# A retention layer feeding a mixture of experts on one core: four-quarter state products, one mask product and a new order inside a chunk

## What is computed

```python
B, H, S, D = 2, 8, 768, 64
gamma = 1.0 - 2.0 ** (-5.0 - arange(H))
for t in range(S):                                   # retention, per batch and head
    state = gamma * state + outer(k[t], v[t])        # D x D
    y[t] = 1/sqrt(D) * (q[t] @ state)
x = y with the heads side by side                    # (B, S, 512)
logits = x @ w_gate; local = sigmoid(x @ w_local)    # 8 experts
e = argmax(logits[s]) if s == 0 or local[s] < 0.5 else e of the token before
out[s] = softmax(logits[s])[e] * (relu(x[s] @ w1[e]) @ w2[e])      # F = 1024
```

## Time and profile before

| | us |
|---|---|
| median of 3 runs | 260.91 (260.75 to 261.23) |
| the profiled execution | 260.31 |
| its span (first to last instruction) | 258.6 |
| PE busy | 248.3 |
| DVE busy | 194.4 |
| ACT busy | 133.6 |
| POOL busy | 62.2 |

### The profile page before, as it was taken

How to read it: one execution, slowest core, us unless ns; L and a number is a source line. 1 busy time by engine, 2 the same in 40 slices (tenths; PEclk the granted TensorE clock), 3 DMA queues, 4 the chain that set the end, 5 groups by cost and what they waited for, 6 DMA issues and landing times.

```text
span 258.6 us, 5040 instructions
## 1 busy us (share of the span) xinstructions
PE 248.3 (96%) x1932; PEld 214.9 (83%) x1932; DVE 194.4 (75%) x426; ACT 133.6 (52%) x254; POOL 62.2 (24%) x57
## 2 busy tenths in 40 slices
PE   7899999999899999999999999999999999999991
PEld 3688888887788888988988898898899889889891
DVE  2445999997986895999798688858869868886700
ACT  1313537537468473557438457545845844764310
POOL 0563343442002423004301600510240061011011
PEclk9999999999999999999999999999999999999998
DMA  6999999962201837556908835771791785440000
GB/s 205 372 380 413 414 411 413 429 246 74 91 0 42 308 124 228 208 175 228 376 18 326 332 150 203 290 310 38 316 392 56 284 314 202 160 203 13 0 38 13
DMA packets 11387, 56.83 MB, mean 220 GB/s; under 512 B 1751, under 2 KB 2135, under 8 KB 9570
## 3 DMA queue, kind: packets, MB, share of 16 engines
q1 hardware_dynamic: 7056, 45.96, 45.8%
q0 software_dynamic: 2560, 7.34, 8.1%
q10 hardware_dynamic: 1746, 3.19, 3.3%
HBM read 50.20 MB, written 7.34 MB: 223 GB/s over the span
## 4 chain that ended last, share of the span: by engine, by line
PE 75%; DVE 12%; DMA 6%; ACT 2%; issue 2%; POOLq 0%; SPq 0%; DVEq 0%
PE ps L1271 18%; PE ps L1290 10%; PE ps L1292 10%; PE ps L1291 10%; PE ps L1273 9%; DMA x_gathered<-x_rows,gather_idx 4%; PE ps L1158 3%; PE ps L1170 3%; PE ps L1251 2%; DVE scores_masked L824 2%; DVE w_split L837 2%; PE ps L1314 2%; PE ps L1203 2%; PE ps L1193 2%; ACT slot_values L549 2%
## 5 line engine op out<-in xcount | busy, mean ns | idle before, releaser
L1271 PE MATMUL ps<-x_sorted_T,w_split 128*128 128x240 f32 (+6 forms) x288 | 84.5, 362 | 0.2 <-DVE x_sorted_T L851 0.2
L1273 PE MATMUL ps<-x_sorted_T,w_split 128*128 128x120 f32 (+6 forms) x288 | 72.7, 252 | 0.0
L844 DVE TENSOR_TENSOR w_split<-w_raw,w_split 128x1024 fp32r<-128x1024 f32 x56 | 66.2, 1220 | 8.2 <-ACT w_split L555 8.2
L555 ACT CAST w_split<-w_raw 128x1024 fp32r<-128x1024 f32 x56 | 55.8, 1041 | 6.5 <-DMA w_raw<-w 6.5
L1271 PEld LDWEIGHTS ps<-x_sorted_T,w_split 128*128 128x128 f32 x288 | 54.1, 188 | 4.2 <-issue 0.7
L1273 PEld LDWEIGHTS ps<-x_sorted_T,w_split 128*128 128x128 f32 x288 | 54.9, 191 | 0.3
L858 DVE TENSOR_REDUCE h_sums<-ps 128x120 f32<-128x240 f32 (+6 forms) x72 | 40.3, 561 | 19.2 <-PE ps L1273 18.4
L565 ACT ACTIVATE hT<-h_sums 128x120 fp32r<-128x120 f32 (+6 forms) x72 | 26.0, 365 | 52.2 <-DVE h_sums L858 52.1
L1290 PE MATMUL ps<-w_split,hT 128*128 128x512 f32 x120 | 48.3, 402 | 0.0
L1292 PE MATMUL ps<-w_split,hT 128*128 128x512 f32 x120 | 47.4, 395 | 0.0
L1291 PE MATMUL ps<-w_split,hT 128*128 128x512 f32 x120 | 47.4, 395 | 0.0
(11 more groups left out here) (146 smaller groups left out, 272.8 us busy)
## 6 DMA issues: line engine op xcount, KB each, us to landing
w_raw<-w SPq DMA_DIRECT2D x14, 2048.0 KB, 9.4
qkv_sb<-qkv SPq DMA_DIRECT2D x22, 512.0 KB, 13.5
w_raw<-w SPq DMA_DIRECT2D x8, 512.0 KB, 16.4
x_rows<-x_rows_sb ACTq DMA_DIRECT2D x12, 256.0 KB, 6.5
qkv_sb<-qkv SPq DMA_DIRECT2D x2, 256.0 KB, 14.5
x_gathered<-x_rows,ident_and_w_router POOLq DMA_INDIRECT x12, 8.5
out<-y_rows,ident_and_w_router POOLq DMA_INDIRECT x12, 5.2
c_route_sb<-c_route SPq DMA_DIRECT2D x1, 152.0 KB, 10.5
```

Of the source, the lines that this page charges most:

```text
L555: nc.scalar.copy(ws[:, par, 0, half, at:at + PIECE], raw[:, half, at:at + PIECE]).then_inc(w_hi_rdy[half], 1)
L844: V.tensor_tensor(ws[:, par, 1, half, at:at + PIECE], raw[:, half, at:at + PIECE], ws[:, par, 0, half, at:at + PIECE].bitcast(fp32), ALU.s ...
L1271: MM(at[:, 0:2 * w].rearrange("p (a t) -> p a t", a=2), ws[:, par, 0, 0, cols], xTs[:, k, :, sub], start=(k == 0), stop=(k == KD - 1), ski ...
L1273: last = MM(at[:, w:2 * w], ws[:, par, 1, 0, cols], xTs[:, k, 0, sub], start=False, stop=(k == KD - 1), skip_group_check=True)
```

## The change

1. `from_state` gives the four 64 by 64 quarters of the array work: row half r takes its head's input as before, and the pair's number n (even or odd) picks the output's partition half. The outputs of the two row halves go to two banks (3 and 4, columns 256 to 511 of each; 0 and 1 for the last chunk). Heads thus stand in another order in x (HEADS), and the host puts the rows of the router and of w1 into the same order.
2. `from_chunk` is cut in two halves by r. The first half (r = 1) goes before `from_state`, the second (r = 0) behind it.
3. `state_products` moves ahead of both, and so waits for the last `state`; `state(m)` on DVE now waits until `from_state(m)` has read the old state (new semaphore `fs_done`).
4. The outputs share bank 3 with the transposed rows, so `from_state(m)` waits until ACT has copied the rows of chunk m - 1 (`xr_ready`). The rows and logits are laid out at steps of 175 columns across banks 2 and 3.
5. `masked` is one instruction of 1024 columns over banks 0 and 1. Just before it DVE raises a new semaphore (`masking`), for which POOL's `k_decayed` of the same chunk waits.
6. ACT's `e0_high` goes behind `logits_out` and `rows_out`. DVE's `e0_low` goes behind `state` in chunks with m % 3 = 2, and behind the router's part at the end of the iteration in the others.

PE's order in iteration m becomes: `qk(m + 1)`, `rows_and_logits(m - 1)`, `to_col`, `state_products(m)`, `from_chunk(m, 1)`, `to_rows`, `table`, `rank`, `from_state(m)`, `from_chunk(m, 0)`. For m = 11 `from_state` and `from_chunk(m, 1)` stand ahead of `rows_and_logits(10)`.

```diff
+HEADS = [0, 2, 4, 6, 1, 3, 5, 7]
+XL_AT, XL_STEP = 25, 175
...
-        y_ps = [bank(n).rearrange("p (n t) -> p n t", n=HP) for n in (4, 1)]
+        xl_ps = bank(2, 2)[:, XL_AT:XL_AT + HP * XL_STEP].rearrange("p (n w) -> p n w", n=HP)
+        y_ps = [bank(n, 2).rearrange("p (r w) -> p r w", r=2)[:, :, 2 * P:4 * P] for n in (3, 0)]
...
+                pool.wait_ge(masking, m + 1)
                 nc.gpsimd.tensor_tensor(
                     kd[:, m % 2, :, :], io[:, s, 2, :, :].rearrange("p n (h d) -> p (n h) d", h=2),
...
             for m in range(NX):
                 g, k = divmod(m, GC)
-                if m in E0_AT:
-                    e0_high(E0_AT[m])
                 if m > 0:
                     logits_out(m - 1)
                     rows_out(m - 1)
+                if m in E0_AT:
+                    e0_high(E0_AT[m])
...
-                for r in range(2):
-                    V.tensor_tensor(sm[:, m % 2, r, :, :], sc_ps[r], masks[:, r, :, :], ALU.mult).then_inc(m_ready, 1)
+                dve.sem_inc(masking, 1)
+                V.tensor_tensor(sm[:, m % 2, :, :, :].rearrange("p r n t -> p (r n t)"), bank(0, 2),
+                                masks[:, :, :, :].rearrange("p r n t -> p (r n t)"), ALU.mult).then_inc(m_ready, 1)
...
                 dve.wait_ge(u_done, b * (NC - 1) + c + 1)
+                if m > 0:
+                    dve.wait_ge(fs_done, b * (NC - 1) + c)
...
-                if m in E0_AT:
-                    e0_low(E0_AT[m])
                 if m % NC < NC - 1:
                     state(m)
+                if m in E0_AT and k == 2:
+                    e0_low(E0_AT[m])
...
+                if m in E0_AT and k < 2:
+                    e0_low(E0_AT[m])
...
+            def y_at(m, r, n):
+
+                return y_ps[m // (NX - 1)][n % 2 * D:n % 2 * D + D, r, n // 2 * P:(n // 2 + 1) * P]
...
                 pe.wait_ge(q_ready, b * (NC - 1) + c)
-                pe.wait_ge(s_ready, b * (NC - 1) + c)
+                if m < NX - 1:
+                    pe.wait_ge(xr_ready, m)
+                else:
+                    pe.wait_ge(s_ready, b * (NC - 1) + c)
...
-            def from_chunk(m):
+            def from_chunk(m, r):
...
+                if m % NC < NC - 1:
+                    state_products(m)
+                if m < NX - 1:
+                    from_chunk(m, 1)
...
-                if m % NC < NC - 1:
-                    state_products(m)
-                from_chunk(m)
+                if m % NC > 0 and m < NX - 1:
+                    from_state(m)
+                from_chunk(m, 0)
```

More of the change, by code:

```diff
@@ L229, in bass_retention_moe_kernel @@
         sc_ps = [bank(r).rearrange("p (n t) -> p n t", n=HP) for r in range(2)]
-        xl_ps = bank(2, 2).rearrange("p (a w) -> p a w", a=2)[:, :, 0:2 * XL].rearrange(
-            "p a (m w) -> p a m w", m=2)
-        y_ps = [bank(n).rearrange("p (n t) -> p n t", n=HP) for n in (4, 1)]
+        xl_ps = bank(2, 2)[:, XL_AT:XL_AT + HP * XL_STEP].rearrange("p (n w) -> p n w", n=HP)
+        y_ps = [bank(n, 2).rearrange("p (r w) -> p r w", r=2)[:, :, 2 * P:4 * P] for n in (3, 0)]
         u_ps = bank(5)[:, 0:HP * D].rearrange("p (n e) -> p n e", n=HP)
@@ L262, in bass_retention_moe_kernel @@
         u_done = sem("u_done")
+        fs_done = sem("from_state_done")
         q_ready = sem("q_decayed_ready")
         m_ready = sem("masked_ready")
+        masking = sem("mask_product_begun")
         s_ready = sem("state_ready")
@@ L580, in _ @@
             act.wait_ge(outer_done, 3)
-            nc.scalar.copy(q_dec[:, :, :], y_ps[0]).then_inc(qdec_ready, 1)
+            nc.scalar.copy(q_dec[:, :, :], bank(4).rearrange("p (n t) -> p n t", n=HP)).then_inc(qdec_ready, 1)
             E0_AT = {3: 0, 4: 1, 5: 2, 7: 3, 8: 4, 10: 5, 11: 6}
@@ L1169, in from_state @@
                         rows = slice(r * D, (r + 1) * D)
-                        MM(y_ps[m // (NX - 1)][rows, n, :], st[rows, n, :], qd[rows, m % 2, n, :],
-                           start=(n == 0), stop=False, skip_group_check=True)
+                        last = MM(y_at(m, r, n), st[rows, n, :], qd[rows, m % 2, n, :],
+                                  start=(n < 2 and (r == 0 or m == NX - 1)), stop=False, skip_group_check=True)
+                last.then_inc(fs_done, 1)
             def state_products(m):
@@ L1183, in state_products @@
                 last.then_inc(u_done, 1)
-            def from_chunk(m):
+            def from_chunk(m, r):
                 s = m % SLOTS
-                pe.wait_ge(kv_in[s], 16 * (m // SLOTS + 1))
-                pe.wait_ge(m_ready, m * 2 + 2)
-                for n in range(HP):
-                    for r in range(2):
-                        rows = slice(r * D, (r + 1) * D)
-                        last = MM(y_ps[m // (NX - 1)][rows, n, :], io[:, s, 3, n, rows], sm[:, m % 2, r, n, :],
-                                  start=(m % NC == 0 and n == 0), stop=True, skip_group_check=True)
-                last.then_inc(y_done, 1)
+                rows = slice(r * D, (r + 1) * D)
+                if r == 1:
+                    pe.wait_ge(kv_in[s], 16 * (m // SLOTS + 1))
+                    pe.wait_ge(m_ready, m + 1)
+                elif m == NC:
+                    pe.wait_ge(xr_ready, m)
+                first = m % NC == 0 or (r == 1 and m < NX - 1)
+                for n in range(HP):
+                    last = MM(y_at(m, r, n), io[:, s, 3, n, rows], sm[:, m % 2, r, n, :],
+                              start=(first and n < 2), stop=True, skip_group_check=True)
+                if r == 0:
+                    last.then_inc(y_done, 1)
             def rows_and_logits(m):
@@ L1202, in rows_and_logits @@
                 for n in range(HP):
-                    last = MM(xl_ps[:, n // 2, n % 2, :], xT[:, m % 2, n, :], idw[:, n, :], start=True, stop=True)
+                    last = MM(xl_ps[:, n, 0:XL], xT[:, m % 2, n, :], idw[:, n, :], start=True, stop=True)
                 last.then_inc(xr_done, 1)
@@ L1337, in _ @@
             pe.wait_ge(qdec_ready, 1)
-            from_chunk(0)
+            from_chunk(0, 1)
+            from_chunk(0, 0)
             state_products(0)
@@ L1343, in _ @@
             qk(2)
+            state_products(1)
+            from_chunk(1, 1)
             from_state(1)
-            state_products(1)
-            from_chunk(1)
+            from_chunk(1, 0)
             for m in range(2, NX):
@@ L1363, in _ @@
                     expert_total()
-                if m % NC > 0 and m < NX - 1:
-                    from_state(m)
+                if m % NC < NC - 1:
+                    state_products(m)
+                if m < NX - 1:
+                    from_chunk(m, 1)
                 if m > GC and m % GC == 1:
@@ L1506, in by_dim, with by_head @@
         return a.reshape(B, HP, 2, NC, P, D).transpose(0, 3, 2, 5, 1, 4).reshape(B * NC * P, HP * P)
+    def by_head(w):
+        return w.reshape(w.shape[:-2] + (H, D, w.shape[-1]))[..., HEADS, :, :].reshape(w.shape)
     def by_token(a):
```

18 lines of the change are left out of this document (9 added, 9 removed).

## The result

The changed kernel takes **263.11 us** (median of 5, 261.72 to 263.58) against 260.75 (260.06 to 261.23) for the kernel before: ratio 1.0073, 95% interval 1.0045 to 1.0101. Two more sets of runs, on two chips, gave 1.0059 (1.0032 to 1.0086) and 1.0052 (1.0019 to 1.0084). It is slower, and 263.11 lies above my range (258.8 to 262.5).

A forecast was written before the change was run, and what follows sets the result against it. PE and DVE together bound the middle of the retention, PE alone the experts. PE's -3.1 us is spent in waits for DVE, leaving -0.2 at the first up: 260.91 - 0.2 = 260.7 us, range 258.8 to 262.5.

The forecast's parts named there:

- The first `up`: First up-projection after the chunks: e0_high(6) waits for rows_and_logits(10), shifting up by +0.4 to -0.5 us; -0.2 taken.
- Four quarters, -0.44 a chunk: PE's from_state: four quarters side by side take 4 steps, 0.44 us in place of 0.88 per chunk.
- PE's 3.1 us are spent in waits for DVE: PE's gain over ten chunks goes into waits: 1.0 at each rank and at expert_total, over 1 at x_lo.
- rival 1: DVE's waits are shorter than added up and PE keeps most of its gain: 258.9 us, at most 257.8; chance 0.22.
- The cut of `from_chunk`, +0.13 a chunk: PE: cutting from_chunk in two adds a change of tile shape, costing 0.13 us per chunk.
- The mask product, -0.6: DVE: one mask product in place of two saves 0.06 us per chunk, 0.6 in all.
- POOL's wait, -0.8: k_decayed waiting for masking moves POOL's work under the mask product, removing a hold of DVE at 37.58: -0.8 us.
- Whether POOL waits for DVE: At chunk 9, expert_total comes at 53.8 as before if POOL waits for an earlier e0_low, 0.9 us earlier if not.
- `state` behind `from_state`, up to 1.0 a time: DVE's state now waits for from_state, 1.0 us later relative to state_products; DVE idles where it has caught up.
- Rival 2: Four quarters do not run at once in from_state: +1.3 to +3.9 us, 262.2 to 264.8; chance 0.13.
- Rival 3: DVE's new idle behind from_state delays mask products until qk waits too: +1.0 us, 261.9; chance 0.13.

The follow-up runs named there:

- d_changed_third: The changed kernel, unaltered, timed again beside the kernel before: 262.78 us, ratio 1.0052.
- the second pair: The changed kernel unaltered, 262.78 us, against the changed kernel with e0_high and e0_low in their former positions, 258.82 us.
- the old places: The changed kernel with e0_high and e0_low put back where the kernel before had them, nothing else: 258.38 us, and 258.82 when repeated.
- d_old_places_again: The changed kernel with e0_high and e0_low put back where the kernel before had them, timed again on another chip: 258.82 us, ratio 0.9913.
- c_chunk_products_whole: The changed kernel with e0_high and e0_low put back and from_chunk in one piece behind from_state: 260.62 us; with two quarters only, 265.35 us.
- a_changed_again: The changed kernel once more, unaltered, timed beside the kernel before: 262.83 us, ratio 1.0059.
- two turned kernels: from_state's loops turned (r outside, n inside): in the changed kernel 263.67 us; in that with e0_high and e0_low put back 259.81 us.

## Why the prediction was wrong

**The step that failed is *The first `up`*.** It put the move of `e0_high(6)` at +0.4 to -0.5 and took -0.2. Measured in the profiled execution of `d_changed_third`: `up` at 70.14 against 68.59 before, +1.55, of which 0.54 is a later start of chunk 0 (6.25 against 5.71). So +1.0. The links of the chain had the lengths that I gave: 2.32 from `rows_and_logits(10)` to `e0_high(6)` (I said 2.3), 1.08 to `e0_low(6)` (1.0), 3.14 to `up` (3.13). What was off:
- `rows_and_logits(10)` came at 63.60 - 0.54 = 63.06 on the base of before, not at 62.6 (0.5). I had counted only PE's gains. In chunk 11 the kernel before already ran `from_state` ahead of `rows_and_logits(10)`, and the new order puts half of `from_chunk(11)` there too, which takes 63.60 - 63.02 = 0.58; my sum had no such term.
- I took a value between my two ends, though my own chain gave +0.4 (0.6).

With 0.1 for the links these make the 1.2 between -0.2 and +1.0. The rest of the distance from 260.7 to 262.8 is not explained by a term of the prediction. 0.54 is the later start of chunk 0, which varies from 5.67 to 6.46 over the traces, and the median stands 1.0 above the profiled execution, against 0.6 before; without the two executions above 267 it would be 0.6 too.

**The larger mistake is in what I compared with.** I followed one order and asked whether its end came later than before. I did not ask what the same change would do with the pieces of expert 0 left in place, and so never saw that this one edit costs 4.0 to 4.5 us in the medians (3.6 in the second pair without the two executions above 267), and 4.1 on the kernel before. From `qk(2)` to the first `up` the traces have 2.5 to 3.4 of it, and 3.96 on the kernel before. It had no rival of its own; the upper end of the range came from rivals 2 and 3, whose mechanisms did not occur.

**Point by point.**
- *Four quarters, -0.44 a chunk*: right. 0.60 where I said 0.57; alone it is worth 0.42 a chunk and 3.6 to 3.9 us (4.7 in the medians, with a late clock in it). The Trainium skill (TensorEngine Tiling (Array Packing), Key Properties) has tiles as independent; the traces agree, with four records beginning within 0.11 us. The prediction took the rule of one bank for each row tile as not contradicted by the earlier trace rows, since the tiles there differ in their columns too. The rule as quoted makes no such exception, and the rows show two row halves at work in one bank at once (two records of 0.32 in 0.33), so here the measurement decides.
- *"PE's 3.1 us are spent in waits for DVE"*: right as a reading of the changed kernel (0.50, 0.60, 0.84 and 1.42 where I said about 1 each), wrong as a cause. Without the move most of these waits are gone, and 1.5 to 2.1 us of PE's gain reach the first `up`. That is rival 1's time (258.9) by a way that it did not name.
- *The cut of `from_chunk`, +0.13 a chunk*: the sign is wrong. It pays 1.8 to 2.2 us, in part (0.7 to 1.3) as cover for the wait for `rows_out`, which I had not seen.
- *The mask product, -0.6*: -0.4 alone, hardly clear of the noise.
- *POOL's wait, -0.8*: right in kind, 1.2 to 1.7, but half a microsecond of it is the hold by `k_decayed` that I meant, the rest a hold by `q_decayed` that it happened to lead to. That is luck of the timing. The wait does not hold POOL until the mask product begins: `k_decayed` starts at 34.05 and the mask at 34.82, with `e0_low` still running.
- *Whether POOL waits for DVE*: it does. `k_decayed` takes 1.65 us beside `e0_low` and 1.04 beside the mask. The Trainium skill (SBUF — State Buffer, SBUF: two separate sides) says that the first to start holds the shared ports and the other waits; both directions are now in the traces. In chunk 8 of `d_changed_third` it went as I said for this case: `q_decayed` (51.59) took 2.05 beside `e0_low`, then held a product of `route_d` to 0.93, and `expert_total` came "as before", 54.48 - 0.54 = 53.9 against 53.8 forecast.
- *`state` behind `from_state`, up to 1.0 a time*: the idle time is there (6.5 us), but a second buffer gives back 0.4 to 0.7, and with the old places it loses 1.0 to 1.5.
- *Rival 2*: refuted by 0.60. *Rival 3*: all waits of `qk` for a mask product make 0.6 us in the profile after; not the cause.

**What stays open.** Why the changed kernel's executions scatter more. In 26 of them 10 had a mean granted clock of 0.990 or less and took 262.85 to 270.89; the other 16 took 261.61 to 263.18, median 262.3. The late pieces are shown as the cause of what is common to all; how the last 0.5 of the median comes about is not shown, since filling PE's waits raised the clock and not the speed. One part of the scatter is not the changed kernel's own: the profiled execution of `d_old_places_again` had its clock full only from 10.2 us and took 260.27, while six of the nine of that program took 258.44 to 259.18. Nor is it shown why `c_chunk_products_whole` with two quarters is 4.5 us slower than before; the waits of `state` and for `rows_out` were only read from the traces.

## What to carry to other kernels

Price each moved piece against the same change without the move, on each engine it passes: a 1 us piece on an engine with 1 us of idle time is free until it is put behind what that engine waits for. The producer's and the consumer's half of such a piece must be placed together, since a late producer turns the consumer's old place into a wait for everything behind it. And before one trusts a "slower", one takes the parts apart: here the other edits (together -2.0 to -2.6 us) were hidden by a bad one; the version with the old places, 258.4 to 258.8, beats both kernels.

## What the hardware showed that I had not expected

- **The clock after the waits.** In `a_changed_again` the granted clock falls to its lower level (1.2 GHz) for 17 us, 2.3 us after the first `up` started. That execution took 268.09, 5.3 above the median. Windows: stretch, length, busy us (instructions) of PE, weight loads, DVE, ACT, POOL; then clock, DMA. That kernel, then the same program in `d_changed_third`:

```profile
66.00:72.50 6.50, 4.12 (x35) 3.33 (x31) 5.34 (x28) 3.27 (x7) 0.00 (x0) 1.00 0.22 82
72.50:89.50 17.00, 17.00 (x75) 16.11 (x76) 8.60 (x39) 9.04 (x30) 1.00 (x1) 0.50 0.06 16
```
```profile
66.00:72.50 6.50, 4.11 (x33) 3.40 (x30) 5.43 (x28) 3.10 (x7) 0.00 (x0) 1.00 0.21 81
72.50:89.50 17.00, 16.39 (x116) 14.28 (x116) 13.19 (x52) 11.89 (x34) 3.76 (x3) 1.00 0.22 74
```

  PE was as busy ahead of it in both (4.12 and 4.11 of 6.5 us), and only one fell. In the fallen stretch PE did 75 records, in the other 116. The old places (15 executions) and the two kernels with products of ones (18) never showed a mean clock at 0.990 or less.
- **An increment runs ahead of the work.** DVE's increment of `masking` stands behind `e0_low` in the program and released POOL at 34.05, while `e0_low` (33.60 to 34.79) was still running.
- **A hold is decided by a few tenths of a microsecond.** `prob_low` took 0.15 at 39.08, 0.26 ahead of POOL's product, and 1.23 at 39.11, 0.16 behind the start of it. An edit that makes DVE or POOL a little earlier can cost 1 us in this way.
- **The order of issue of the four quarters did not matter to the block**: with either nesting of the loops four records began within 0.04 us, and the block took 0.60 or 0.61. The medians of the two turned kernels were higher even so (0.8 and 1.0 to 1.4), which is not explained.
